# An unused tensor of 128 bytes per partition is placed in SBUF ahead of the token and hidden-value tensors

## The reference

```
w = softmax(weight_gen, over 7 taps)                  # 2 x 4096 tokens, 8 heads
x = sum over taps of w[tap] * x shifted by tap        # 8192 x 192
h = max(x @ w_in, 0);  x = (h*h) @ w_out              # 192 -> 2048 -> 192
h = x @ w_in2;  g = h * clip(h + 3, 0, 6) / 6;  out = g @ w_out2
```

## Time and profile before

| | |
|---|---|
| median of 3 runs | 1164.6 us (1164.34 to 1167.81) |
| the profiled execution's own time | 1168.12 us |
| its span, first to last instruction | 1166.3 us |
| PE busy | 1153.4 us, 99% |
| PEld busy | 1147.6 us, 98% |
| DVE busy | 924.5 us, 79% |
| ACT busy | 675.9 us, 58% |
| granted clock of TensorE | 1.00 |
| DMA | mean 36 GB/s |

### The profile page before, as it was taken

How to read it: one execution, slowest core, us unless ns; L and a number is a source line. 1 busy time by engine, 2 the same in 40 slices (tenths; PEclk the granted TensorE clock), 3 DMA queues, 4 the chain that set the end, 5 groups by cost and what they waited for, 6 DMA issues and landing times.

```text
span 1166.3 us, 26723 instructions
## 1 busy us (share of the span) xinstructions
PE 1153.4 (99%) x10412; PEld 1147.6 (98%) x10412; DVE 924.5 (79%) x1054; ACT 675.9 (58%) x772; POOL 3.7 (0%) x11
## 2 busy tenths in 40 slices
PE   7999999999999999999999999999999999999998
PEld 7999999999999999999999999999999999999997
DVE  8889797887968879697786978879688796976565
ACT  6887645556555565645556455564555556555554
POOL 1000000000000000000000000000000000000000
PEclk9999999999999999999999999999999999999999
DMA  7211003020030200202011020200302002010001
GB/s 214 79 63 53 5 2 76 4 66 12 0 74 4 70 9 13 61 4 72 6 49 29 0 74 4 65 14 0 74 4 69 10 13 61 0 38 3 1 15 28
DMA packets 78190, 41.93 MB, mean 36 GB/s; under 512 B 55952, under 2 KB 72462, under 8 KB 78156
## 3 DMA queue, kind: packets, MB, share of 16 engines
q1 hardware_dynamic: 78156, 41.45, 13.8%
HBM read 30.00 MB, written 11.40 MB: 36 GB/s over the span
## 4 chain that ended last, share of the span: by engine, by line
PE 94%; ACT 2%; DVE 1%; DMA 1%; issue 1%; SPq 0%; DVEq 0%; ACTq 0%
PE h_ps L910 45%; PE y_ps L921 30%; PE y_ps L930 20%; DMA stage<-in_moe_w_in_dram 1%; ACT hid L444 1%; ACT hid L449 1%; ACT win L431 0%; ACT hid_hi L457 0%; DVE acc L610 0%; DVE hid_lo L711 0%; SPq L292 0%; DVE prod L632 0%; DVE wout L677 0%; DVE hid L700 0%; SPq L302 0%
## 5 line engine op out<-in xcount | busy, mean ns | idle before, releaser
L910 PE MATMUL h_ps<-xt,win 64*128 64x512 f32 (+1 forms) x4860 | 1068.9, 379 | 1.0 <-DVE wout L677 0.9
L910 PEld LDWEIGHTS h_ps<-xt,win 64*128 64x128 f32 x4860 | 826.6, 184 | 2.0 <-DVE wout L677 1.3
L921 PE MATMUL y_ps<-hid_hi,wout 64*128 64x512 f32 (+1 forms) x2160 | 562.5, 379 | 0.7 <-DVE win L677 0.5
L460 ACT ACTIVATE hid_hi<-hid 128x1024 fp32r<-128x1024 f32 (+1 forms) x244 | 256.4, 1051 | 316.8 <-DVE hid L702 155.5
L711 DVE TENSOR_TENSOR hid_lo<-hid,hid_hi 128x1024 fp32r<-128x1024 f32 (+1 forms) x270 | 313.2, 1160 | 143.0 <-ACT hid_hi L460 137.8
L921 PEld LDWEIGHTS y_ps<-hid_hi,wout 64*128 64x128 f32 x2160 | 385.2, 184 | 1.9 <-DVE win L677 0.7
L921 PE MATMUL y_ps<-hid_lo,wout 64*128 64x512 f32 (+1 forms) x1080 | 323.1, 378 | 1.0 <-DVE hid_lo L711 1.0
L930 PE MATMUL y_ps<-hid_lo,wout 64*128 64x512 f32 (+1 forms) x1080 | 322.9, 378 | 0.0
L930 PE MATMUL y_ps<-hid_hi,wout 64*128 64x512 f32 (+1 forms) x1080 | 322.8, 378 | 0.0
L921 PEld LDWEIGHTS y_ps<-hid_lo,wout 64*128 64x128 f32 x1080 | 194.6, 184 | 1.7 <-DVE hid_lo L711 1.4
L930 PEld LDWEIGHTS y_ps<-hid_hi,wout 64*128 64x128 f32 x1080 | 194.6, 184 | 0.2
(11 more groups left out here) (87 smaller groups left out, 325.8 us busy)
## 6 DMA issues: line engine op xcount, KB each, us to landing
xwin<-in_x_dram SPq DMA_DIRECT2D x14, 960.0 KB
by_feature<-stage SPq DMA_DIRECT2D x52, 96.0 KB, 2.0
out_dram<-outs SPq DMA_DIRECT2D x240, 16.0 KB, 1.5
out_dram<-outs SPq DMA_DIRECT2D x240, 8.0 KB, 1.4
stage<-by_feature SPq DMA_DIRECT2D x13, 256.0 KB, 3.0
stage<-in_moe_w_out_dram SPq DMA_DIRECT2D x8, 384.0 KB, 5.8
stage<-in_moe_w_in_dram SPq DMA_DIRECT2D x4, 512.0 KB, 6.9
stage<-in_moe_w_in_dram SPq DMA_DIRECT2D x8, 256.0 KB, 6.2
```

Source lines behind the costliest of these rows:

```text
L460: act.activation(hi, hid[:, slot, :, 0:width], ACT.Copy).then_inc(hi_done, 1)
L910: return pe.matmul(h_ps[:, s % 2, t, 0:tokens.stop - tokens.start], win[layer][r, wn, cols], src[r, xn, tokens], start=bool(rows) and n in ...
L921: return pe.matmul(ps[:, 0, tokens], wout[layer][r, tile, w_cols], src, start=bool(rows) and s == 0 and n == 0, stop=not rows and s == STE ...
```

## The change

One tensor that nothing reads or writes is put between `prod` and `xt`. It takes 32 numbers of 4 bytes in each partition, and every tensor behind it moves up by 128 bytes.

```
         prod = sb("prod", [P, 2, J * D])
 
 
+
+        sb("gap", [P, Q])
         xt = [sb(f"xt{n}", [P, 4, N], fp32r) for n in range(2)]
         hid = sb("hid", [P, 2, PAIR, N])
         hid_hi = sb("hid_hi", [P, 2, PAIR, N], fp32r)
```

## The result

The changed kernel takes 1138.92 us (median of 4 runs, 1138.48 to 1139.29); the kernel before, run beside it, 1166.2 us (1164.34 to 1169.11). The ratio is 0.9764, 95% interval 0.9739 to 0.9788: 27.3 us less, where 1133 us and a gain of 31.9 had been forecast. The spans are 1137.5 and 1166.3 us. The 45 executions of the kernel before that the runs of this case hold fall into two groups, 13 from 1163.8 to 1165.8 us and 32 from 1167.8 to 1170.3 us, with none between; its trace is of one of the longer group (1168.12 us), and the changed kernel has one group only.

The account below looks back on a forecast made before the run. The prediction took the rate of TensorE's own stream as the bound. Terms of 30.0 and 1.9 us summed to 31.9 us, taking the median from 1164.6 to about 1133 us, with an 8-in-10 range of 1129 to 1168 us.

Parts of the forecast that it names:

- Term 1: Matmuls of 512 columns in row groups: 4540 a group, each giving back 6.6 ns, 30.0 us in all.
- Term 2: Matmuls of 256 columns in row groups: about 570 a group, each 3.4 ns faster in proportion, 1.9 us gained.
- Cover of VectorE and ScalarE: Steady part: tightest hand-over, `hid_lo` to its matmul, has 0.92 us; faster steps take 0.25 us, so TensorE should not wait.
- DMAs: 480 small DMAs out of `outs`: hidden up to the last one, costed at nothing, at most some tenths of a microsecond.
- Nothing: Row-group matmuls: the 6.6 ns come from having 64 rows, so no gain and 1164.6 us; chance 0.33.
- Slower: Moving operands off multiples of 256 cover nine 256-byte blocks instead of eight, costing 23.0 us: 1188 us; chance 0.15.
- Part of it: Row-group matmul distance falls only to a middle value; at half of the 6.6 ns, 16 us gained, 1149 us; chance 0.15.
- Built elsewhere: Chip addresses shifted by 128 against the built program: moving operands still reach `win0`'s remainder, first term unchanged; no separate chance.

## Why the prediction was right

**The bound.** TensorE's own stream sets the time, right: 99% busy before and after, no idle time in the steady part, and the whole gain is the distance between its starts.

**Term 1, 30.0 us.** Right in size and by its own reading: 30.07 us measured between the first matmul of 512 columns and the tail, 226.7 ns where the `win0` stretch had suggested it. This compares with an execution of the longer group. If the shorter ones of the kernel before go at the 232.4 ns that was seen with everything moved, an estimate for them is 4540 x 5.7 ns = 25.9 us. Its weak point, two stretches that differed in two things, is settled by the run with `win0` shifted: the address makes nearly all of it. That it is the equality with the weights and not the place of the moving operand was left open in the prediction; moving everything (ratio 0.9991) and moving the weights alone (0.9746) decide it.

**Term 2, 1.9 us.** Wrong in sign. The proportion was carried from 512 to 256 columns without a row; 120.0 ns were measured where 118.7 had been, which costs 0.7 us over the 570 matmuls of a group. With this term at -0.7 and 0.5 us for the start the sum is 28.8 us, which is what the span lost.

**From the span to the median.** The span was forecast at 1134.4 us and came to 1137.5; the 3.1 us between are term 2 and the start. The median was forecast at about 1133 us and came to 1138.92, and the rest of that miss lies in the base: the 31.9 us had been worked out from an execution of 1168.12 us and were taken from a median of 1164.6 us, of three executions of which two belonged to the shorter group.

**Cover of VectorE and ScalarE.** Right, but thinner than worked out. The tightest hand-over I found after, in the timelines of DVE and PE:

```profile
287.20 1.22 DVE L713 TENSOR_TENSOR hid_lo<-hid,hid_hi 128x1024 fp32r<-128x1024 f32 x1
```

```profile
288.79 0.39 PE L923 MATMUL y_ps<-hid_lo,wout 64*128 64x512 f32 x1
```

`hid_lo` ends at 288.42 and is used at 288.79: 0.37 us, where 0.92 less 0.25 had left 0.67. Their durations did not change (`hid_lo` is 1.22 us in both), so the order in which VectorE gets to it must have; that a convolution operation falls elsewhere is my reading, which no run shows. By these numbers a further gain of the same size would leave nothing of it, as an estimate. DMAs: nothing, as costed.

**Rules of the pages.** That weight loads take no bandwidth from the running matmul (the Trainium skill, "TensorE: Matmul & The Clock Gate", Step-by-step) would have meant no gain. The measurement decides against its use here: 6.6 ns a matmul hang on how weights and moving operand lie to each other, and moving the weights alone takes them away (ratio 0.9746). The 16-byte cachelines (the Trainium skill, "SBUF — State Buffer", Specifications) don't foresee a difference between multiples of 128 either; here the period is 256 bytes.

**The rivals.** *Nothing* fell with the runs of 226.7 ns. *Slower*, by blocks of 256 bytes, fell: equal remainders are as fast at 128 as at 0, though at 128 nine blocks are touched. *Part of it* did not occur. *Built elsewhere* is not needed: what counts is the difference of two addresses, so the words of the change (multiples of 256, counted from `win0`) and the built addresses (off them) describe the same equality.

**What stays open.** Why equality helps: that the reads of weights and moving operand disturb each other by their places in SBUF would fit the smaller price with short loads, but not the slower equal case with them, nor the 13.3 ns that remain above 512 columns at 2.4 GHz. No run shows how these reads go. Why unequal remainders have two rates, 233.3 and about 232 ns, is open too.

## What to carry to other kernels

When a stream of matmuls has no waits and yet goes slower than its columns at the granted clock, look at the distance of starts in stretches whose operands lie elsewhere; two rates for the same shape are a lead. Where, as here, 4-byte operands of 512 columns have a weight load ahead of every matmul, try the same remainder by 256 bytes for weights and all moving operands, and read the addresses from the built program: the first tensor here begins at byte 16512, not at a multiple of 256. Match all moving operands, not one of two, and test narrow matmuls apart.

## What was not expected of the hardware

- Equal remainders give 226.7 ns for 512 columns, differences of 32, 64 and 128 bytes all give 233.3 (232.4 in one execution at 128): a step, not a slope.
- For 256 columns the order is another, and it doesn't follow the difference alone: in 16 us 280 matmuls at a difference of 64 bytes, 275 at 128, 271 at equality, but 272 with the moving operands 32 bytes short of the weights' remainder and 279 with them 32 bytes past it.
- With equal remainders, halving the weight columns of 22 of 38 matmuls (loads of 132 instead of 184 ns) made the distance longer, 229.5 against 226.7 ns, in one run.
